# Order of high and low halves around the start of a fused attention and feed-forward kernel: values behind the transposed probabilities, the sixth pair's scores one slot later, the ninth weight behind slot 3

## Chip, cores and metric

One core of a Trainium2 chip. The metric is the device time of the core in microseconds (us), less is better. One launch computes everything.

## The reference

Attention with pooled keys and values (8 batches, 8 heads, 576 positions, head size 64), whose output is laid out as 4608 tokens of 512 and goes through two feed-forward layers (512 to 2048 to 512 each), all in float32:

```python
k_p = k.reshape(B, H, Sp, 8, D).mean(axis=3)
v_p = v.reshape(B, H, Sp, 8, D).mean(axis=3)
attn = softmax(q @ k_p.T / sqrt(D))          # cut
x = attn @ v_p                                # -> 4608 x 512
h = x @ w_in1
g = where(h >= 1, h, where(h <= -1, 0, (h + 1) ** 2 / 4))
x = g @ w_out1
r = maximum(x @ w_in2, 0)
out = (r * r) @ w_out2
```

## The kernel before, in words

Every float32 product is made of three products in a faster type: each operand is split in a high half, rounded on ScalarE, and a low half, the difference, made on VectorE or GpSimd. high x high, high x low and low x high are summed in PSUM. So each operand has two preparing steps (names ending in `_high` and `_low`).

The first part of the kernel goes over 12 chunks of 384 tokens and, in each, over 4 pairs of heads: 48 pairs, called a. For each pair TensorE makes `scores(a)` (L696 on, matmuls L709), VectorE subtracts the row maximum (`below`, L1240 and L1244), ScalarE takes the exponential (`exps`, L954), VectorE normalises (`normal`, L1253 to L1267), TensorE transposes (`transposes`, L722 and L725), ScalarE and VectorE copy out a high and a low half of the transposed probabilities (`probabilities` L960 and L963, `probabilities_low` L1272 and L1276), TensorE multiplies them with the values (`values`, L743 to L746), and the result is split again (`tokens_high`, `tokens_low`, L1283).

Meanwhile the first feed-forward product runs: chunk c has 16 tiles of the hidden dimension, slot g = 16 c + j, one `hidden(g)` of 12 matmuls (L754) in each. Its activation is made by ScalarE (L1073, called relu here, and L1076, the square) and VectorE (L1408, semaphore `g_made`), and stored by SyncE to DRAM through a ring of four tiles `g_st`. relu(g) waits for the store of g - 4. Slots 0 to 3 of the first chunk are done with raw float32 operands (`first_hidden`, L784); hidden(4) is the first split one.

The values of a batch and pair of heads, m, are folded by GpSimd (`fold` L579, `values` L585, L589, L593, giving `v_bd`), ScalarE makes the high half (`values_high`, L989), GpSimd the low ones (`values_low`, L601 and L604). `spread_keys` (L571) places the pooled keys. `v_bd` is one buffer: the last step of `values(m)` waits until `values_low(m - 1)` is done. The 16 tiles of the first weight are split by `weights_high(j)` (L993) on ScalarE and `weights_low(j)` on GpSimd (L610), tiles 4 and 5 on VectorE (L1288).

No planner orders the work: each engine has a list written out by hand, and within it each step waits on semaphores. In the slots a step of a pair stands where `pairs_at(g, step)` puts it (L220 on): steps 0 to 6 are scores; exps and below; normal; transposes; probabilities; values; tokens. Pairs 4 to 7 have a first slot each (1, 4, 7, 9), later ones every fourth slot. In a slot, TensorE does hidden, values, transposes, scores; ScalarE probabilities, tokens_high, relu and square, exps; VectorE probabilities_low, below, tokens_low, normal, and the activation. What GpSimd does before the slots is a straight list (L664 to L686). On ScalarE, `values_high(5..7)` and `weights_high(8..15, 0..3)` stand behind given slots (L1115 to L1123). Pair 5's `scores` also wait for `g_made` 4, since slot 3 used the bank of its output. `hidden(g)` waits for g_made of g - 3 or g - 2 and, in its first round, for its weight's low half.

Before the slots, ScalarE ends its list with exps(4), tokens_first(3) (L969), values_high(4), tokens_high(3); VectorE ends it with weights_low(4), tokens_low(1), weights_low(5), tokens_low(2), tokens_low(3), and then comes the activation of slot 0 and normal(4).

The other parts (a fast product of the block kind for the second, third and fourth feed-forward matrices, L886 and L909) are 75% of the time and not touched.

Of the kernel before, what the change touches and what calls it, by code (L numbers as in the profile page):

```python
# [19 lines left out]
def attention_then_two_ffns(nc, q, k, v, v_rest, w_in1, w_out1, w_in2, w_out2, out, g_dram, y_dram, s_dram):  # L20
# [12 lines left out]


    NC, HP, _, H = q.shape
    B = k.shape[0]
    NF, _, D = w_in1.shape
    S = NC * H // B
    G = S // POOL
# [24 lines left out]
    with ExitStack() as ctx:  # L64
# [139 lines left out]
        def pv_bank(a):  # L204

            return tr_ps[:, P:P + H] if a >= REST_APART and a % 2 else o_ps[:, 0:H]
# [13 lines left out]
        def done(m):  # L220

            return HP * ((S * (m // HP + 1) - 1) // H) + m % HP + 1

        def pairs_at(g, step):

            first = {4: 1, 5: 4, 6: 7, 7: 9}

            def taken_at(a):  # L230
                if a < REST_APART:
                    return first[a] + step
                return 4 * (a - 5) + step + (4 if step > 4 and a % 2 == 0 else 0)

            return [a for a in range(HP, PAIRS) if taken_at(a) == g and (a > HP or step > 2)]
# [17 lines left out]
        def wi_count(j):  # L253

            return (j - FIRST) % NF + 1
# [304 lines left out]
        def _(pool):  # L560
# [5 lines left out]
            def spread_keys(m):  # L566

                pool.wait_ge(k_pooled, m + 1)
                if m >= KRING:
                    pool.wait_ge(s_full, done(m - KRING))  # L570
                pool.tensor_tensor(kT[:, m % KRING, :].rearrange("p (h n) -> p h n", h=2),  # L571
                                   k_pool[m % 2][:, :].unsqueeze(1).broadcast_to([P, 2, G]),
                                   head[:, :].unsqueeze(2).broadcast_to([P, 2, G]), ALU.mult).then_inc(k_ready, 1)

            def fold(m):

                raw = v_raw[m % VRAW]
                pool.wait_ge(v_in[m % VRAW], 64 * (m // VRAW + 1))
                pool.tensor_tensor(raw[:, :, 0:4], raw[:, :, 0:4], raw[:, :, 4:8], ALU.add).then_inc(v_half, 1)  # L579

            def values(m):

                raw = v_raw[m % VRAW]
                pool.wait_ge(v_half, m + 1)
                pool.tensor_tensor(raw[:, :, 0:2], raw[:, :, 0:2], raw[:, :, 2:4], ALU.add).then_inc(v_quarter, 1)  # L585
                pool.wait_ge(v_quarter, m + 1)
                if m:
                    pool.wait_ge(v_spread, m)
                pool.tensor_tensor(v_pool[:, :, :], raw[:, :, 0], raw[:, :, 1], ALU.add).then_inc(v_pooled, 1)  # L589
                pool.wait_ge(v_pooled, m + 1)  # L590
                if m:
                    pool.wait_ge(v_ready, m)
                pool.tensor_tensor(v_bd[:, :, :].rearrange("p m (h d) -> p m h d", h=2),  # L593
                                   v_pool[:, :, :].unsqueeze(2).broadcast_to([P, 2, 2, Dh]),
                                   mask[:, :, :].unsqueeze(3).broadcast_to([P, 2, 2, Dh]), ALU.mult)\
                    .then_inc(v_spread, 1)

            def values_low(m):
                pool.wait_ge(v_hi_ready, m + 1)
                vh, rows = v_hi[m % KRING], slice(64, REST_ROWS)  # L600
                pool.tensor_tensor(v_lo[m % KRING][:, :], v_bd[:, 0, :], vh[:, 0, :].bitcast(F32), ALU.subtract)\  # L601
                    .then_inc(v_low_made, 1)
                pool.wait_ge(v_low_made, m + 1)
                pool.tensor_tensor(vh[rows, 1, :], v_bd[rows, 1, :], vh[rows, 1, :].bitcast(F32), ALU.subtract)\  # L604
                    .then_inc(v_ready, 1)
                pool.wait_ge(v_ready, m + 1)

            def weights_low(j):
                pool.wait_ge(wi_hi_ready, wi_count(j))
                pool.tensor_tensor(wi_lo[j][:, :], wi_raw[j][:, :], wi_hi[j][:, :].bitcast(F32), ALU.subtract)\  # L610
                    .then_inc(wi_ready, 1)
# [44 lines left out]
            for m in range(HP):  # L656
                if m == 1:
                    spread_keys(3)
                fold(m + 1)
                if m in (0, 2):  # L660
                    spread_keys(m + 2)
                values_low(m)
                values(m + 1)
            weights_low(6)  # L664
            values_low(4)
            weights_low(7)
            spread_keys(5)
            fold(5)
            values(5)
            weights_low(8)  # L670
            spread_keys(6)
            values_low(5)
            weights_low(9)
            fold(6)
            values(6)
            weights_low(10)
            spread_keys(7)
            values_low(6)
            weights_low(11)
            fold(7)  # L680
            values(7)
            weights_low(12)
            weights_low(13)
            values_low(7)
            weights_low(14)
            weights_low(15)  # L686
            pool.wait_ge(h_full, FIRST)
            for j in range(FIRST):
                weights_low(j)
# [258 lines left out]
        def _(act):  # L948
            copy = nc.scalar.activation

            def exps(a):
                act.wait_ge(s_below, a + 1)
                probs = prob[a % 2][:, :, :]
                copy(probs, probs, ACT.Exp, scale=Dh ** -0.5 / POOL).then_inc(s_exp, 1)  # L954
# [11 lines left out]
            def tokens_first(a):  # L966

                act.wait_ge(pv_full, a + 1)
                copy(x_first[:, a, :], o_ps[:, 0:H], ACT.Copy).then_inc(x_first_ready, 1)  # L969

            def tokens_high(a):
                c = a // HP
                if c == 0:
                    act.wait_ge(x_first_ready, a + 1)
                    copy(x_hi[0][:, a, :], x_first[:, a, :], ACT.Copy).then_inc(x_hi_ready, 1)
                    return
                act.wait_ge(pv_full, a + 1)
                if c == 1:
                    act.wait_ge(h_full, FIRST)
                    act.wait_ge(x_ready, HP)  # L980
                else:
                    act.wait_ge(h_full, NF * (c - 1))
                copy(x_hi[c % 2][:, a % HP, :], pv_bank(a), ACT.Copy).then_inc(x_hi_ready, 1)

            def values_high(m):
                act.wait_ge(v_spread, m + 1)
                if m >= KRING:
                    act.wait_ge(pv_full, done(m - KRING))
                copy(v_hi[m % KRING][:, :, :], v_bd[:, :, :], ACT.Copy).then_inc(v_hi_ready, 1)  # L989

            def weights_high(j):
                act.wait_ge(weight_in[j], 16)
                copy(wi_hi[j][:, :], wi_raw[j][:, :], ACT.Copy).then_inc(wi_hi_ready, 1)  # L993
# [116 lines left out]
            weights_high(7)  # L1110
            exps(4)
            tokens_first(3)
            values_high(4)
            tokens_high(3)
            for g in range(SLOTS):  # L1115
                slot(g)
                for m, at_slot in ((5, 4), (6, 7), (7, 10)):
                    if g == at_slot:
                        values_high(m)
                for j in {1: (8,), 4: (9,), 5: (10,), 6: (11, 12), 7: (13,), 8: (14,), 9: (15,), 10: (0,), 11: (1, 2),  # L1120
                          12: (3,)}.get(g, ()):
                    weights_high(j)

            for n in range(6, ALL + 4):
# [96 lines left out]
        def _(dve):  # L1221
# [57 lines left out]
            def tokens_low(a):  # L1279
                c, hp = divmod(a, HP)  # L1280
                dve.wait_ge(x_hi_ready, a + 1)
                raw = pv_bank(a) if c else x_first[:, hp, :]
                vec.tensor_tensor(x_lo[c % 2][:, hp, :], raw, x_hi[c % 2][:, hp, :].bitcast(F32),  # L1283
                                  ALU.subtract).then_inc(x_ready, 1)

            def weights_low(j):
                dve.wait_ge(wi_hi_ready, wi_count(j))
                vec.tensor_tensor(wi_lo[j][:, :], wi_raw[j][:, :], wi_hi[j][:, :].bitcast(F32), ALU.subtract)\  # L1288
                    .then_inc(wi_ready_first, 1)
# [172 lines left out]
            probabilities_low(3)  # L1462
            weights_low(4)
            tokens_low(1)
            weights_low(5)
            tokens_low(2)
            tokens_low(3)
            for g in range(-4, SLOTS):
                slot(g)

# [182 lines left out]
```

## Time and profile before

| what | value |
|---|---|
| median of 3 runs | 1573.02 us (1572.12 to 1574.9) |
| the profiled execution's own time | 1574.91 us |
| its span in the profile | 1573.1 us |
| TensorE matmul busy | 1563.8 us (99%) |
| VectorE, ScalarE, GpSimd busy | 1126.4, 831.2, 248.0 us |
| TensorE clock granted | 0.9 or more of full speed in every slice |

The profiler's span runs from the first to the last instruction; all times in the views count from its start. PE is TensorE, DVE VectorE, ACT ScalarE, POOL GpSimd, SP SyncE. In a timeline a row is an instruction, or several alike merged, with its start, its length, what it writes and reads, and in brackets the time that the engine stood idle before it and who released it. A line such as L610 is the line of a helper in the kernel, so tiles are told apart by their order.

### The profile page before, as it was taken

What the parts mean: (1) busy time and instruction counts of PE and PEld (TensorE: products, weight loads), DVE (VectorE), ACT (ScalarE), POOL (GpSimd) and SP (SyncE); (2) the same over time, 40 slices, a digit from 0 to 9 for tenths busy, and PEclk for the clock granted to TensorE, in tenths of its full rate; (3) what the DMA queues carried; (4) which work ended last, traced back from release to release, by engine and by line L of the source; (5) the groups of instructions that cost most, each with busy time, mean ns of one, the idle gap of its engine ahead of it and who ended that gap; (6) DMA issues with size and microseconds to landing.
All of it is one profiled execution on the core that took longest, in us unless ns stands there. A gap on an engine that the chain in (4) does not pass through costs nothing.

```text
span 1573.1 us, 25372 instructions
## 1 busy us (share of the span) xinstructions
PE 1563.8 (99%) x9160; PEld 1545.1 (98%) x9160; DVE 1126.4 (72%) x1823; ACT 831.2 (53%) x1488; POOL 248.0 (16%) x356
## 2 busy tenths in 40 slices
PE   8999999999999999999999999999999999999999
PEld 6999999999999999999999999999999999999999
DVE  7666666667666877877879767667667986876874
ACT  5766668666667544443445654344356643443442
POOL 7655338735500000000000000000000000000000
PEclk9999999999999999999999999999999999999999
DMA  9367479566537444245244642442448645245231
GB/s 292 109 225 226 166 220 326 183 210 228 190 112 244 153 161 152 94 157 164 83 156 169 220 160 101 141 161 103 139 159 289 194 149 195 74 144 186 91 116 41
DMA packets 173950, 262.79 MB, mean 167 GB/s; under 512 B 16640, under 2 KB 153856, under 8 KB 173824
## 3 DMA queue, kind: packets, MB, share of 16 engines
q1 hardware_dynamic: 173824, 261.16, 50.3%
q8 instruction: 73, 1.20, 0.3%
q14 instruction: 53, 0.43, 0.1%
HBM read 154.14 MB, written 106.95 MB: 166 GB/s over the span
## 4 chain that ended last, share of the span: by engine, by line
PE 93%; DVE 3%; ACT 1%; POOL 1%; DMA 1%; issue 1%; SPq 0%; DVEq 0%; POOLq 0%; ACTq 0%
PE bank L886 42%; PE bank L754 24%; PE bank L909 21%; PE bank L709 2%; PE bank L722 1%; DVE gf L1327 1%; DVE b L1320 1%; PE bank L746 1%; PE bank L743 1%; PE bank L744 1%; PE bank L745 1%; DMA f_raw<-moe_w_out 0%; DVE f_lo L1295 0%; ACT pT_rest L963 0%; POOL v_raw L579 0%
## 5 line engine op out<-in xcount | busy, mean ns | idle before, releaser
L886 PE MATMUL bank<-gf,f_hi 128*128 128x384 f32 x2688 | 682.7, 334 | 0.5 <-DVE u_b L1337 0.4
L886 PEld LDWEIGHTS bank<-gf,f_hi 128*128 128x128 f32 x2688 | 485.5, 188 | 1.3 <-DVE u_b L1337 0.9
L886 PE MATMUL bank<-gf,f_lo 128*128 128x384 f32 x1344 | 449.1, 334 | 0.0
L1022 ACT ACTIVATE gf<-b 128x768 fp32r<-128x768 f32 x336 | 278.6, 845 | 264.4 <-PE bank L886 174.1
L1327 DVE TENSOR_TENSOR gf<-b,gf 128x768 fp32r<-128x768 f32 x336 | 314.5, 952 | 43.3 <-ACT gf L1022 43.3
L909 PE MATMUL bank<-xf,w_hi 128*128 128x384 f32 x1344 | 341.6, 335 | 1.0 <-ACT c_st L1154 0.7
L754 PE MATMUL bank<-x_hi,wi_hi 128*128 128x384 f32 x752 | 259.9, 346 | 0.8 <-DVE g_st L1408 0.8
L886 PEld LDWEIGHTS bank<-gf,f_lo 128*128 128x128 f32 x1344 | 252.3, 188 | 0.0
L754 PE MATMUL bank<-x_hi,wi_lo 128*128 128x384 f32 x752 | 252.1, 335 | 0.0
L754 PE MATMUL bank<-x_lo,wi_hi 128*128 128x384 f32 x752 | 252.1, 335 | 0.0
L909 PEld LDWEIGHTS bank<-xf,w_hi 128*128 128x128 f32 x1344 | 242.2, 188 | 2.6 <-ACT c_st L1154 1.7
L909 PE MATMUL bank<-xf,w_lo 128*128 128x384 f32 x672 | 224.6, 334 | 0.0
L1408 DVE SCALAR_TENSOR_TENSOR g_st<-g_st,bank 128x384 f32<-128x384 f32 x192 | 106.0, 553 | 116.6 <-ACT g_st L1076 116.0
L1073 ACT ACTIVATE g_st<-bank,half_sb 128x384 f32<-128x384 f32 x192 | 111.5, 581 | 146.6 <-PE bank L754 142.6
L1320 DVE TENSOR_TENSOR b<-b,b 128x768 f32<-128x768 f32 x192 | 182.3, 952 | 0.0
L754 PEld LDWEIGHTS bank<-x_hi,wi_hi 128*128 128x128 f32 x752 | 141.5, 188 | 1.4 <-DVE g_st L1408 1.4
L754 PEld LDWEIGHTS bank<-x_lo,wi_hi 128*128 128x128 f32 x752 | 141.5, 188 | 0.0
L754 PEld LDWEIGHTS bank<-x_hi,wi_lo 128*128 128x128 f32 x752 | 141.2, 188 | 0.0
L909 PEld LDWEIGHTS bank<-xf,w_lo 128*128 128x128 f32 x672 | 126.2, 188 | 0.0
L1076 ACT ACTIVATE g_st<-g_st 128x384 f32<-128x384 f32 x192 | 101.0, 526 | 6.1
L1154 ACT ACTIVATE c_st<-bank 128x384 f32<-128x384 f32 x48 | 23.3, 486 | 99.6 <-PE bank L909 99.6
L1502 DVE TENSOR_TENSOR u<-bank,p 128x384 f32<-128x384 f32 x48 | 26.7, 557 | 44.0 <-PE bank L909 36.3
(105 smaller groups left out, 1484.5 us busy)
## 6 DMA issues: line engine op xcount, KB each, us to landing
b<-g_dram SPq DMA_DIRECT2D x192, 384.0 KB, 4.4
g_dram<-g_st SPq DMA_DIRECT2D x192, 192.0 KB, 2.4
g_dram<-c_st SPq DMA_DIRECT2D x192, 192.0 KB, 1.9
s_dram<-su_s SPq DMA_DIRECT2D x24, 512.0 KB, 2.9
k_raw<-k SPq DMA_DIRECT2D x32, 288.0 KB, 3.7
q_sb<-q SPq DMA_DIRECT2D x48, 192.0 KB, 3.1
y_dram<-o_st SPq DMA_DIRECT2D x48, 192.0 KB, 2.1
x_raw<-y_dram SPq DMA_DIRECT2D x24, 384.0 KB, 5.3
```

The source lines that it names most:

```text
L709: last = mm(s_ps[a % 2][m0 - t * P:m1 - t * P, t * KEYS:(t + 1) * KEYS], q_sb[a % QRING][:, m0:m1], kT[:, m % KRING, :], start=True, stop= ...
L754: last = mm(h_bank(g)[:, 0:H], w[j][:, cols], x[:, kt, :], start=kt == 0 and n == 0, stop=kt == KT - 1 and n == 2)
L886: last = mm(dst[:, 0:H], w[:, 2 * i + kt, cols], x[:, half, kt, :], start=q_ < 3 and i == 0 and kt == 0 and h == 0, stop=q_ >= 4 and i == ...
L909: last = mm(dst[:, 0:H], w[:, form, cols], x[:, half, kt, :], start=i < 3 and kt == 0 and h == 0, stop=i >= 4 and kt == 1 and h == 2, skip ...
L1022: copy(gf[layer][r % GRING][:, 0], unit_source(n)[:, 2 * i:2 * i + 2, :], ACT.Copy).then_inc(gf_hi, 1)
L1073: copy(g_st[g % GST][:, :], h_bank(g)[:, 0:H], ACT.Relu, bias=half_sb[:, 0:1], scale=0.5)\
L1076: copy(g_st[g % GST][:, :], g_st[g % GST][:, :], ACT.Square).then_inc(act_ready, 1)
L1154: copy(c[:, :], xa_ps[n % 2][:, 0:H], ACT.Relu).then_inc(r11_made, 1)
L1320: vec.tensor_tensor(out_[:, rows, :], first[:, rows, :], other[:, rows, :], ALU.subtract)\
L1327: vec.tensor_tensor(halves[:, 1], unit_source(n)[:, 2 * i:2 * i + 2, :], halves[:, 0].bitcast(F32), ALU.subtract).then_inc(gf_ready, 1)
L1408: vec.scalar_tensor_tensor(h[:, :], h[:, :], 1.0, h_bank(g)[:, 0:H], ALU.min, ALU.max)\
L1502: vec.tensor_tensor(u2[n % 2][:, :], ya_ps[n % 2][:, 0:H], p1[n % 2][:, :], ALU.add).then_inc(u2_made, 1)
```

## The change

It moves steps in three of the hand-written lists and changes one entry of the slot table; no instruction is added or removed.

- TensorE: scores(5) stand in slot 5 instead of slot 4.
- ScalarE: tokens_high(3) before values_high(4). values_high(5), (6), (7) behind slots 5, 8, 11 instead of 4, 7, 10. weights_high(8), (9) behind slot 3 (were behind 1 and 4), (13) behind 8 (was 7), (0) behind 11 (was 10), (1), (2) behind 12 (were 11), (3) behind 13 (was 12).
- VectorE: weights_low(5) behind tokens_low(3) instead of ahead of tokens_low(2).
- GpSimd: values_low(4) before weights_low(6); weights_low(9) before values_low(5); values_low(6) behind fold(7), and values_low(7) behind the last weight.

```diff
@@ pairs_at
             def taken_at(a):
                 if a < REST_APART:
-                    return first[a] + step
+
+                    return first[a] + step + (a == HP + 1 and step == 0)
...
@@ GpSimd
                 values_low(m)
                 values(m + 1)
+            values_low(4)
             weights_low(6)
-            values_low(4)
             weights_low(7)
             spread_keys(5)
             fold(5)
             values(5)
             weights_low(8)
             spread_keys(6)
+            weights_low(9)
             values_low(5)
-            weights_low(9)
             fold(6)
             values(6)
             weights_low(10)
             spread_keys(7)
-            values_low(6)
             weights_low(11)
             fold(7)
+            values_low(6)
             values(7)
-            weights_low(12)
-            weights_low(13)
+            for j in range(12, NF):
+                weights_low(j)
             values_low(7)
-            weights_low(14)
-            weights_low(15)
@@ ScalarE
             tokens_first(3)
+            tokens_high(3)
             values_high(4)
-            tokens_high(3)
             for g in range(SLOTS):
                 slot(g)
-                for m, at_slot in ((5, 4), (6, 7), (7, 10)):
+                for m, at_slot in ((5, 5), (6, 8), (7, 11)):
                     if g == at_slot:
                         values_high(m)
-                for j in {1: (8,), 4: (9,), 5: (10,), 6: (11, 12), 7: (13,), 8: (14,), 9: (15,), 10: (0,), 11: (1, 2),
-                          12: (3,)}.get(g, ()):
+                for j in {3: (8, 9), 5: (10,), 6: (11, 12), 8: (13, 14), 9: (15,), 11: (0,), 12: (1, 2),
+                          13: (3,)}.get(g, ()):
                     weights_high(j)
@@ VectorE
             tokens_low(1)
-            weights_low(5)
             tokens_low(2)
             tokens_low(3)
+            weights_low(5)
```

## Rows read from the trace of the kernel before

**Rows 1.** The page's first part: engine, busy us (share), instructions.
```profile
PE 1563.8 (99%) x9160; PEld 1545.1 (98%) x9160; DVE 1126.4 (72%) x1823; ACT 831.2 (53%) x1488; POOL 248.0 (16%) x356
```

**Rows 2.** Waits of TensorE, whole run: us in total, times, longest.
```profile
PE bank L722 <- DVE prob L1267: 1.5, 5, 0.5
...
PE bank L754 <- DVE g_st L1408: 0.8, 1, 0.8
```

**Rows 3.** Timeline of TensorE, 30 to 63 us: start, length, what.
```profile
30.03 3.59 PE L784 MATMUL bank<-x_first,wi_raw 128*128 128x384 f32 x10
34.43 0.44 PE L754 MATMUL bank<-x_hi,wi_hi 128*128 128x384 f32 x1 [0.81 <-DVE g_st L1408]
...
36.62 0.27 PE L722 MATMUL bank<-ident,prob 128*128 128x128 f32 x1
...
37.52 1.32 PE L709 MATMUL bank<-kT,q_sb 128*128 128x144 f32 x8
...
46.27 0.33 PE L722 MATMUL bank<-ident,prob 128*128 128x128 f32 x1 [0.27 <-DVE prob L1267]
...
60.98 0.34 PE L754 MATMUL bank<-x_hi,wi_lo 128*128 128x384 f32 x1
61.38 0.36 PE L743 MATMUL bank<-pT_hi,v_hi 128*128 128x192 f32 x1
...
62.98 0.33 PE L722 MATMUL bank<-ident,prob 128*128 128x128 f32 x1 [0.46 <-DVE prob L1267]
```

**Rows 4.** The chain that ended last: start, time on the chain, what.
```profile
95.28 6.25 PE bank L754 x36
```

**Rows 5.** Timeline of VectorE, 30 to 43 us.
```profile
30.54 1.10 DVE L1288 TENSOR_TENSOR wi_lo<-wi_raw,wi_hi 128x512 fp32r<-128x512 f32 x1
...
31.56 2.35 DVE L1283 TENSOR_TENSOR x_lo<-x_first,x_hi 128x384 fp32r<-128x384 f32 x2
...
33.83 0.54 DVE L1408 SCALAR_TENSOR_TENSOR g_st<-g_st,bank 128x384 f32<-128x384 f32 x1
...
42.64 0.61 DVE L1240 TENSOR_REDUCE top<-bank 128x6 f32<-128x432 f32 x1
```

**Rows 6.** Tile wi_lo, 0 to 70 us: ns min/median/max, first and last start.
```profile
L610 POOL TENSOR_TENSOR wi_lo<-wi_raw,wi_hi x14: 1274/1290/1715, 31.0 to 65.8; 128x512 fp32r<-128x512 f32 x14
L1288 DVE TENSOR_TENSOR wi_lo<-wi_raw,wi_hi x2: 693/896/1098, 29.2 to 30.5; 128x512 fp32r<-128x512 f32 x2
```

**Rows 7.** Timeline of GpSimd, 30 to 57 us.
```profile
30.27 0.81 POOL L593 TENSOR_TENSOR v_bd<-v_pool,mask 128x256 f32<-128x256 f32 x1
31.05 1.72 POOL L610 TENSOR_TENSOR wi_lo<-wi_raw,wi_hi 128x512 fp32r<-128x512 f32 x1
32.73 0.77 POOL L601 TENSOR_TENSOR v_lo<-v_bd,v_hi 128x128 fp32r<-128x128 f32 x1
...
52.54 0.73 POOL L585 TENSOR_TENSOR v_raw<-v_raw 128x256 f32<-128x256 f32 x1
...
54.46 2.54 POOL L610 TENSOR_TENSOR wi_lo<-wi_raw,wi_hi 128x512 fp32r<-128x512 f32 x2
```

**Rows 8.** Timeline of ScalarE, 30 to 57 us.
```profile
30.23 0.49 ACT L969 ACTIVATE x_first<-bank 128x384 f32<-128x384 f32 x1 [0.29 <-PE bank L746]
...
31.12 0.42 ACT L989 ACTIVATE v_hi<-v_bd 128x256 fp32r<-128x256 f32 x1 [0.40 <-POOL v_bd L593]
...
38.03 0.58 ACT L1073 ACTIVATE g_st<-bank,half_sb 128x384 f32<-128x384 f32 x1 [1.46 <-DMA g_dram<-g_st]
...
39.28 0.42 ACT L989 ACTIVATE v_hi<-v_bd 128x256 fp32r<-128x256 f32 x1
...
40.13 0.47 ACT L960 ACTIVATE pT_hi<-bank 128x384 fp32r<-128x384 f32 x1
...
53.00 0.56 ACT L954 ACTIVATE prob<-prob 128x432 f32<-128x432 f32 x1 [1.30 <-DVE prob L1244]
...
56.52 0.58 ACT L1073 ACTIVATE g_st<-bank,half_sb 128x384 f32<-128x384 f32 x1 [0.52 <-PE bank L754]
```

## The prediction

> **What bounds the kernel now.** I read the page first: TensorE is busy for 1563.8 us of a span of 1573.1 us [rows 1]. So nearly all that a new order can bring is the 9 us in which TensorE stands still, and the next question is where. The waits of TensorE over the whole run answer it: five waits for the normalised probabilities, 1.5 us, and one of a hidden product for the feed-forward activation on VectorE, 0.8 us [rows 2], are the long ones that the change can reach. The timeline of TensorE puts them in the first 63 us [rows 3]; three of the five lie before 30 us, where nothing changes. A matmul of this product is recorded 0.33 us long while the next one follows 0.174 us later (36 in 6.25 us [rows 4]), so an idle time in the timeline is about 0.16 us shorter than the time that the issue was held up. I count hold-ups:
> - hidden(4) starts at 34.43; the raw products before it end at 33.62, so it could start at 33.46: 0.97 us.
> - scores(5) starts at 37.52; the six transposes before it (0.11 us each from 36.62) are issued by 37.28: 0.24 us. It waits for g_made 4.
> - transposes(5) at 46.27, idle 0.27: 0.43 us.
> - values(6) at 61.38, after a matmul issued at 60.98: 0.23 us.
> - transposes(7) at 62.98, idle 0.46: 0.62 us.
> That is 2.49 us, 0.16% of the span. Nothing else in the time that the change touches holds TensorE.
>
> **Part 1: the start (tokens_high(3) before values_high(4) on ScalarE, tokens_low(2), (3) before weights_low(5) on VectorE, values_low(4) before weights_low(6) on GpSimd).** No instruction is added; the gain or loss is in who waits. In the rows VectorE's weights_low(5) takes 1.10 us and the two x_lo behind it 2.35 us, before the activation of slot 0 starts at 33.83 [rows 5]; alone the first of these takes about 0.6 to 0.69, as its sister [rows 6]. On GpSimd the same window holds v_bd to 31.08, weights_low(6) of 1.72 us (its median is 1.29 [rows 6]), then v_lo of 0.77 [rows 7]. The ends alternate: v_bd 31.08, DVE 31.64, POOL 32.77, DVE about 33.1, POOL 33.5, DVE 33.91. Each VectorE instruction that reads two SBUF tensors takes its turn with GpSimd's. So VectorE's start is late mostly by one long turn of GpSimd, weights_low(6).
> New order: x_first(3) ends at 30.72, v_bd at 31.08 [rows 8, 7]. ScalarE does x_hi(3) at about 30.75 to 31.25 (it is as large as x_first, 0.49) and v_hi(4) right behind, done at 31.57 where it was 31.54: no loss. GpSimd has nothing until then, 0.5 us idle. VectorE: x_lo(2) in its turn 31.04 to 31.54, x_lo(3) next to 32.04 (GpSimd asks at 31.64, just too late), v_lo to 32.45, weights_low(5) to 33.0, then the activation at about 32.95 instead of 33.83, whose square from ScalarE is there at 32.6. hidden(4) then starts at 33.55: **0.88 us earlier**. Bounds: if GpSimd's v_lo gets in ahead of x_lo(3), VectorE ends its three 0.46 us later, 0.42 us gained; the upper bound is the 0.97 us. I take 0.88 because the request of VectorE is 0.1 us ahead by the rows.
> Another reading of the same stretched rows is that two engines share the port and both run slower; VectorE then gains only what GpSimd's idle 0.5 us gives back, about 0.55 us. The Trainium skill ("SBUF — State Buffer", section "SBUF: two separate sides") says that the port pair shared by VectorE and GpSimd is an exclusive lock held for a whole instruction, not a split of bandwidth: by that rule the term is 0.88, or 0.42 if the order of arrival flips. With it the trace agrees, in its alternating ends.
> GpSimd ends weights_low(7) and values(5) about 0.45 us later than now. Covered: hidden(6) and hidden(7), which need weights 6 and 7, start near 39.6 and 42.6, some 5 us behind those.
>
> **Part 2: scores(5) one slot later.** TensorE does transposes(4), hidden(5), scores(5), hidden(6). The matmuls are the same. scores(5) no longer stands right behind g_made 4: **0.24 us gained**. What is late next: below(5) on VectorE. It stands behind probabilities_low(4) and started at 42.64 [rows 5], 4.61 behind relu(4); by part 3 that becomes 37.15 + 4.61 - 0.85 = 40.9, and scores(5) is done at about 39.6. Cost nothing; without that cover at most the 1.3 us that scores(5) took [rows 3]. Weights 8 and 9 made on ScalarE behind slot 3 lie in its wait for a store, 1.46 us idle before 38.03 [rows 8]: two of 0.52.
> SyncE issues no transfer at another place. Its loads of q wait for earlier scores only; the next one that counts scores(5) is in slot 9.
>
> **Part 3: values_high(5), weight 9 gone from behind slot 4.** They took 39.28 to 40.13, 0.85 us, right ahead of the copies of the transposed probabilities of pair 4 [rows 8]. The chain relu(4), square, probabilities(4), probabilities_low(4), below(5), exps(5), normal(5), transposes(5) ran from 38.03 to 46.27, 8.24 us; now 7.39. relu(4) is released by the store of activation 0, 4.20 us behind the start of that activation (33.83 to 38.03). From 32.95 that is 37.15, so the probabilities are there at 44.54. TensorE, from hidden(4) at 33.55, needs 46.27 - 34.43 less the 0.24 and 0.43 held up, 11.17 us: it comes at 44.72. The hold-up goes, **0.43 us**, with 0.2 us to spare. Bound: if the store lands at its old time, it is 45.42, a wait of 0.7.
>
> **Part 4: the same for pairs 6 and 7.** values_high(7) and weight 0 leave their place between exps(7) and probabilities(6). The chain from relu(10) at 56.52 to transposes(7) at 62.98 is 6.46 us, less 0.85 is 5.61; TensorE without its hold-ups needs 62.98 - 56.52 - 0.62 - 0.23 = 5.61. So **0.85 us** go, by a hair. If one late copy stays, 0.2 to 0.4 us come back.
>
> **Part 5: GpSimd behind values_high(6).** weights_low(12) now stands behind values_low(6) and values(7). transposes(5) to exps(6) was 46.27 to 53.00, 6.73; 0.84 less for values_high(6) and weight 13: exps(6) starts at 44.72 + 5.89 = 50.6. v_hi(6) is then done at 51.5, values_low(6) (1.0) at 52.6, values(7) (52.54 to 54.46 [rows 7]) at 54.5, weights_low(12) (1.29) at 55.8. hidden(12) starts 12 x 0.174 ahead of 61.15, at 59.07 now, 57.5 then. Spare 1.7 us (it was 3.3). Cost nothing.
>
> **Sum:** 0.88 + 0.24 + 0.43 + 0.85 = 2.4 us. Two of the terms are ties, so I take 2.1 to 2.2. Behind 75 us TensorE waits for other engines only at places that are counted from its own pace, so a head start is kept. The profiled execution took 1574.91 us with a span of 1573.1, and is 1.9 above the median of the three runs, 1573.02. Its span should become 1571.0; against the median that is 1570.9.
>
> **Rivals.**
> - *A half gain.* The lock goes to GpSimd (0.42 for 0.88) or the store lands late (a wait of 0.7 at transposes(5)), or the tie at transposes(7) falls wrong. For it: margins of 0.1 and 0.2 us, DMA traffic in this stretch. Against: the rows put each on the good side. Gain 0.8 to 1.6, 1571.4 to 1572.2.
> - *No change at all.* The waits are only moved: hidden(4) starts earlier, but the probabilities of pairs 5 and 7 are as late as they were (46.2 and 62.9), so TensorE waits there for what it won, and the end is the same: 1573.0. It takes both stores and copies to stay put; relu(4) hanging on a DMA speaks for it, 0.85 us of ScalarE work taken away against it.
> - *Slower: GpSimd's chain becomes the bound at hidden(12).* Place: weights_low(12) behind values_low(6) and values(7), all behind v_hi(6). From v_hi(6) to the end of weights_low(12) is 4.3 us by part 5, so hidden(12) waits as soon as v_hi(6) is done after 53.2. The old run had hidden(12) at 59.07 and lost 0.85 us behind it, so the kernel is slower than before once hidden(12) starts after 59.92, v_hi(6) done after 55.6. If v_hi(6) comes only where v_hi(7) came, done at about 58.4, hidden(12) starts at 62.7, 2.8 us past that point: 1575.8. For it: GpSimd is busy nearly throughout this stretch and now waits for two more copies. Against: v_hi(6) would have to be 4 us behind my count.
> - *The change does more:* a chain freed early makes TensorE's small hold-ups elsewhere in the first 75 us smaller as well. All the waits that are listed there are counted above, so little is left: 1569.8.
>
> **How the numbers follow.** A difference under 0.2%, 3.1 us, can't be told from no change in this kernel. Forecast (gain 1.7 to 2.6) 0.6; half gain 0.2; no change 0.08; slower than before 0.05; more 0.07. Three runs of the same kernel lie 2.8 us apart, so a median may be 1 us off. That gives the forecast case itself about one chance in eight to be read as over 3.1 us faster; with the last case, faster is 0.13; slower by over 3.1 us is 0.03; within is 0.84. The range takes in the half gain and most of no change, and 1.4 us below for the measurement: 1569.5 to 1573.3.
>
> **What would show it.** In the timeline of TensorE: hidden(4) at 33.5 to 33.9 with an idle time under 0.2; transposes(4) followed by hidden(5) and scores(5) without a hold-up; transposes(5) near 44.8 and transposes(7) near 60.7 with none, and hidden(16) some 2.4 us earlier than now. On VectorE three short turns ahead of an activation near 33.0. On GpSimd an idle time of 0.5 us before the v_lo of pair 4. It is wrong if relu(4) still starts at 38.0, if hidden(12) waits for a weight from GpSimd, or if waits of another pair appear.

## The result and the profile after

| | before | after |
|---|---|---|
| median | 1573.04 us (1572.12 to 1574.9, 22 runs) | 1570.65 us (1569.9 to 1572.69, 22 runs) |
| ratio | | 0.9987, 95% interval 0.9981 to 0.9993 |
| span of the profiled execution | 1573.1 us | 1568.5 us |

The kernel is 2.4 us faster, 0.15%, with the interval clear of no change. The spans are 4.6 us apart; the runs below show that some 2.1 of that isn't the change's.

TensorE's busy time in the page of the kernel after (line numbers from here on are those of the kernel that a row comes from: in the kernels made from the new one they are one lower on ScalarE, VectorE and TensorE and one higher on GpSimd and SyncE):

```profile
span 1568.5 us, 25371 instructions
...
PE 1562.2 (100%) x9160; PEld 1545.7 (99%) x9160; DVE 1125.6 (72%) x1823; ACT 831.1 (53%) x1488; POOL 247.7 (16%) x356
```

Its waits over the whole run. The first row is a wait within the first 2 us, the same before. The one for the activation (0.8 us in [rows 2]) is gone; that for the probabilities is 0.9 in 4 instead of 1.5 in 5, and all that is left of it lies before 30 us. At transposes(7) the starts below still show a hold-up of some 0.1 us, too short for an idle time:

```profile
PE bank L804 <- DVE head L1428: 1.1, 1, 1.1
PE bank L721 <- DVE prob L1266: 0.9, 4, 0.3
```

The timeline of TensorE after, at the places of [rows 3]: hidden(4), transposes(4), scores(5), transposes(5), values(6), transposes(7), and hidden(16), which started at 71.86 before. None has an idle time in brackets:

```profile
33.48 0.44 PE L753 MATMUL bank<-x_hi,wi_hi 128*128 128x384 f32 x1
...
35.67 0.27 PE L721 MATMUL bank<-ident,prob 128*128 128x128 f32 x1
...
38.42 1.25 PE L708 MATMUL bank<-kT,q_sb 128*128 128x144 f32 x8
...
44.59 0.30 PE L721 MATMUL bank<-ident,prob 128*128 128x128 f32 x1
...
59.44 0.25 PE L742 MATMUL bank<-pT_hi,v_hi 128*128 128x192 f32 x1
...
60.44 0.33 PE L721 MATMUL bank<-ident,prob 128*128 128x128 f32 x1
...
69.40 0.42 PE L753 MATMUL bank<-x_hi,wi_hi 128*128 128x384 f32 x1
```

The timelines of VectorE, GpSimd and ScalarE after, for [rows 5], [rows 7] and [rows 8]. The three x_lo take 2.17 us together, weights_low(5) 0.94, and the activation of slot 0 starts at 32.87 (33.83 before). GpSimd now does the two steps of values_low(4) first (L602, L605) and weights 6 and 7 after them, in 2.54 us together, no longer stretched; weight 12 starts at 54.72 (the row holds weights 12 to 15). relu(4) starts at 37.38, the high halves of pairs 5 and 6 at 42.69 and 51.25.

```profile
29.77 2.17 DVE L1282 TENSOR_TENSOR x_lo<-x_first,x_hi 128x384 fp32r<-128x384 f32 x3
31.87 0.94 DVE L1287 TENSOR_TENSOR wi_lo<-wi_raw,wi_hi 128x512 fp32r<-128x512 f32 x1
32.87 0.55 DVE L1407 SCALAR_TENSOR_TENSOR g_st<-g_st,bank 128x384 f32<-128x384 f32 x1
```

```profile
31.64 0.62 POOL L602 TENSOR_TENSOR v_lo<-v_bd,v_hi 128x128 fp32r<-128x128 f32 x1 [0.58 <-ACT v_hi L988]
32.34 0.78 POOL L605 TENSOR_TENSOR v_hi<-v_bd,v_hi 32x128 fp32r<-32x128 f32 x1
33.20 2.54 POOL L611 TENSOR_TENSOR wi_lo<-wi_raw,wi_hi 128x512 fp32r<-128x512 f32 x2
...
54.72 5.03 POOL L611 TENSOR_TENSOR wi_lo<-wi_raw,wi_hi 128x512 fp32r<-128x512 f32 x4
```

```profile
37.38 0.58 ACT L1072 ACTIVATE g_st<-bank,half_sb 128x384 f32<-128x384 f32 x1 [0.42 <-DMA g_dram<-g_st]
...
42.69 0.40 ACT L988 ACTIVATE v_hi<-v_bd 128x256 fp32r<-128x256 f32 x1
...
51.25 0.40 ACT L988 ACTIVATE v_hi<-v_bd 128x256 fp32r<-128x256 f32 x1
```

**How the runs are compared.** Whole runs of one kernel spread over 0.8 to 4.1 us and the parts are worth less, so I compare places in the timeline of TensorE. (One of the later executions of the kernel before took 2590.92 us; the medians don't feel it.) The last block of raw products starts at 29.66 to 30.56 us in the profiles (30.03 in [rows 3]), so all is counted from its start to the start of hidden(16): D. It splits in four: raw block to hidden(4); to transposes(5); to transposes(7); to hidden(16).

| kernel | to hidden(4) | to transposes(5) | to transposes(7) | to hidden(16) | D | median us |
|---|---|---|---|---|---|---|
| before | 4.40 | 11.84 | 16.71 | 8.88 | 41.83 | 1573.04 |
| before again (c_before) | 4.65 | 11.85 | 16.71 | 8.86 | 42.07 | 1572.71 |
| after | 3.47 | 11.11 | 15.85 | 8.96 | 39.39 | 1570.65 |
| e_start | 3.46 | 12.92 | 16.71 | 8.87 | 41.96 | 1573.22 |
| e_slots | 4.43 | 11.12 | 15.84 | 8.95 | 40.34 | 1571.43 |
| e_scores | 4.41 | 11.87 | 16.72 | 8.86 | 41.86 | 1572.77 (1 run) |
| e_start5 | 3.47 | 11.50 | 18.21 | 8.86 | 42.04 | 1573.57 |
| e_pool | 4.38 | 11.13 | 15.84 | 8.95 | 40.30 | 1571.29 |
| e_dve | 3.47 | 11.42 | 15.89 | 8.97 | 39.75 | 1570.61 (1 run) |
| e_act | 3.88 | 11.12 | 15.89 | 8.98 | 39.87 | 1570.39 (1 run) |
| e_noscores | 3.79 | 11.42 | 15.84 | 8.98 | 40.03 | 1571.08 |
| e_vh6 | 3.56 | 11.48 | 22.22 | 8.81 | 46.07 | 1576.51 |
| e_vh6_9 | 3.47 | 11.11 | 16.67 | 9.07 | 40.32 | 1571.64 |
| e_forms | 3.47 | 11.15 | 15.88 | 8.97 | 39.47 | 1570.73 |

In D the change is worth 2.44 us, as much as in the medians (2.39).

### The profile page after: what moved, and what is told of

The parts are those of the page before. It is cut to its first block, busy times and chain, and to the rows that moved or that the text cites. A ratio compares the mean times of both kernels' runs of the same rounds, so it can differ in the third digit from the quotient of the medians.

```text
span 1568.5 us, 25371 instructions
## 1 busy us (share of the span) xinstructions
PE 1562.2 (100%) x9160; PEld 1545.7 (99%) x9160; DVE 1125.6 (72%) x1823; ACT 831.1 (53%) x1488; POOL 247.7 (16%) x356
## 4 chain that ended last, share of the span: by engine, by line
PE 96%; DVE 2%; issue 0%; ACT 0%; DMA 0%; DVEq 0%; ACTq 0%
PE bank L885 42%; PE bank L753 25%; PE bank L908 22%; PE bank L708 2%; PE bank L721 1%; DVE gf L1326 1%; DVE b L1319 1%; PE bank L745 1%; PE bank L742 1%; PE bank L743 1%; PE bank L744 1%; PE bank L783 0%; DVE f_lo L1294 0%; PE bank L791 0%; PE bank L724 0%
## 5 line engine op out<-in xcount | busy, mean ns | idle before, releaser
L1352 DVE TENSOR_TENSOR o_st<-bank,u_b 128x384 f32<-128x384 f32 x48 | 26.7, 557 | 41.8 <-PE bank L885 41.0
```

The source lines that it names most:

```text
L1352: vec.tensor_tensor(o_st[layer][o % OUTS][:, :], src[:, 0:H], more[:, :], ALU.add)\
```

## Experiments

### The kernel before, once more, and the parts

**c_before**, no edit.

> The kernel before, unchanged, as a control. The profiles of the two kernels are 4.6 us apart while the medians are 2.4 apart; the first product is 2.5 us ahead at its end, and the other 2.1 us lie between the first and the last matmul of L909 (867.6 to 1219.2 before, 865.2 to 1214.6 after), where ScalarE waits for f_raw from DRAM. Theory A (it belongs to that one execution): this stretch takes 349 to 350 us here and the time is 1573.0. Theory B (it belongs to the old order): 351.6 us again. Both expect hidden(16) to start at 71.9 and a ratio of 1.000.

Measured: ratio 1.0001 (0.9992 to 1.001). The stretch of L909 took 349.1 us (867.9 to 1217.0). The rows of that line, the kernel after first, then the control (count, ns min/median/max, first and last start):

```profile
L908 PE MATMUL bank<-xf,w_hi x1344: 334/334/440, 865.2 to 1214.6; 128*128 128x384 f32 x192
```

```profile
L909 PE MATMUL bank<-xf,w_hi x1344: 334/334/334, 867.9 to 1217.0; 128*128 128x384 f32 x192
```

Theory A holds: of all fourteen profiles of this study the stretch is 349.1 to 349.6 in twelve, 350.3 in e_start's and 351.6 in the first one of the kernel before. So some 2.1 us of the 4.6 belong to that execution, not to its order. The control shows one thing more, which I had not looked for. ScalarE's timeline in it:

```profile
37.20 0.58 ACT L1073 ACTIVATE g_st<-bank,half_sb 128x384 f32<-128x384 f32 x1 [0.40 <-DMA g_dram<-g_st]
...
39.52 0.42 ACT L989 ACTIVATE v_hi<-v_bd 128x256 fp32r<-128x256 f32 x1 [1.18 <-POOL v_bd L593]
```

Here the store landed early and relu(4) started at 37.20 instead of 38.03. It helped nothing: values_high(5) then stood 1.18 us waiting for GpSimd, and transposes(5) came as late as ever (11.85). In this execution GpSimd, not the store, set that chain; e_scores and e_start below show the same.

**e_start**, the start alone:

```diff
 ScalarE   +tokens_high(3) ahead of values_high(4)
 VectorE   +weights_low(5) behind tokens_low(3)
 GpSimd    +values_low(4) ahead of weights_low(6)
 (on the kernel before)
```

> The start alone on the kernel before: tokens_high(3) ahead of values_high(4), weights_low(5) behind tokens_low(3), values_low(4) ahead of weights_low(6). My theory: activation of slot 0 at 32.9, hidden(4) at 33.5 (0.95 earlier); relu(4) near 37.2, so with values_high(5) and weight 9 still in its chain (8.24 us) transposes(5) comes near 45.4 and TensorE waits about 0.5 to 0.7 there; the waits at values(6) and transposes(7) stay. hidden(16) starts at 71.1 to 71.2 instead of 71.9, time 1572.3. Rival 'the parts are independent': the full 0.95 is kept, hidden(16) at 70.9.

Measured: hidden(4) 0.94 us earlier, as expected, and nothing of it left at hidden(16). The ratio is 1.0001 (0.9991 to 1.001). It is worse than my theory: from hidden(4) to transposes(5) takes 12.92, 1.08 more, so all 0.94 are given back. TensorE, then ScalarE:

```profile
34.00 0.44 PE L754 MATMUL bank<-x_hi,wi_hi 128*128 128x384 f32 x1
...
37.69 1.32 PE L709 MATMUL bank<-kT,q_sb 128*128 128x144 f32 x8 [0.68 <-DVE g_st L1408]
...
46.92 0.33 PE L722 MATMUL bank<-ident,prob 128*128 128x128 f32 x1 [0.36 <-DVE prob L1267]
```

```profile
39.93 0.42 ACT L989 ACTIVATE v_hi<-v_bd 128x256 fp32r<-128x256 f32 x1 [0.97 <-POOL v_bd L593]
```

scores(5) still stands behind g_made 4 (idle 0.68), and values_high(5) waits 0.97 us for `v_bd`, which GpSimd, idle 0.6 us at the new start, makes no earlier than before. Both theories fell; e_start5 below takes up the cause.

**e_slots**, all but those three edits:

```diff
 ScalarE   -tokens_high(3) ahead of values_high(4)
 VectorE   -weights_low(5) behind tokens_low(3)
 GpSimd    -values_low(4) ahead of weights_low(6)
 (on the kernel after)
```

> All of the change but the start. My theory: hidden(4) stays at 34.4; scores(5) has no hold-up (0.24), transposes(5) comes near 45.6 without one (0.43), the 0.85 at values(6) and transposes(7) go but for 0.15. hidden(16) starts at 70.4 to 70.5, 1.4 to 1.5 us earlier than before; time 1571.6. Rival 'the moves pay only with the early start': waits stay at transposes(5) and (7), hidden(16) at 71.5 or later.

Measured: D 40.34, 1.49 us less than before; ratio 0.9989 (0.998 to 0.9998). As expected: hidden(4) stays, the hold-ups at transposes(5) and behind go (11.12 and 15.84, the values of the kernel after). So the slots pay by themselves, the start only with them: 0.95 on top of the slots, nothing alone.

**e_scores**, scores(5) alone:

```diff
-                    return first[a] + step
+                    return first[a] + step + (a == HP + 1 and step == 0)
 (on the kernel before)
```

> Only scores(5) one slot later. My theory: the 0.24 hold-up of scores(5) goes, but transposes(5) hangs on relu(4) and the copies behind it and stays at 46.3, with an idle time of about 0.5 instead of 0.27; net nothing, hidden(16) at 71.9. Rival 'scores(5) one slot later gives its 0.24': hidden(16) at 71.6. Rival 'it delays below(5) and so the pair': transposes(5) later than 46.3.

Measured: the expected result. D 41.86; the wait moves to transposes(5), idle 0.36 us instead of 0.27. The reason that I gave is not what the run shows: relu(4) started at 37.55, 0.5 us earlier than before, and transposes(5) came no earlier, because values_high(5) waited for `v_bd` again. TensorE, then ScalarE:

```profile
46.26 0.33 PE L722 MATMUL bank<-ident,prob 128*128 128x128 f32 x1 [0.36 <-DVE prob L1267]
```

```profile
39.28 0.42 ACT L989 ACTIVATE v_hi<-v_bd 128x256 fp32r<-128x256 f32 x1 [0.59 <-POOL v_bd L593]
```

### Where the start's 0.94 us comes from, and the rival

**e_pool**:

```diff
-            values_low(4)
             weights_low(6)
+            values_low(4)
 (GpSimd, on the kernel after)
```

> The kernel after, but with weights_low(6) ahead of values_low(4) on GpSimd again. Measured as D, from the start of the last block of raw products (30.0) to the start of hidden(16): 41.8 before, 39.4 after. Theory 'whole turns': VectorE's three instructions and GpSimd's alternate, x_lo(2), weights_low(6), x_lo(3), v_lo, weights_low(5); the activation of slot 0 starts near 34.35 where it was 32.9, even later than before (33.8), hidden(4) near 34.95, D 40.9. Rival 'both share the port': the same instructions run at the same time as before the change, activation at 33.8, hidden(4) 34.4, D 40.3. Rival 'GpSimd's order is free': 32.9, D 39.4.

Measured: 4.38 us from the raw block to hidden(4), as before the change; D 40.30, ratio 0.9989 (0.9979 to 0.9998). Without GpSimd's one swap the whole gain of the start is gone (the swap alone was not run). The number that came is that of "both share the port", though the rows look like turns. VectorE, then GpSimd (all about 0.4 later than in the kernel after, as the raw block is):

```profile
30.20 3.24 DVE L1282 TENSOR_TENSOR x_lo<-x_first,x_hi 128x384 fp32r<-128x384 f32 x3
33.36 0.94 DVE L1287 TENSOR_TENSOR wi_lo<-wi_raw,wi_hi 128x512 fp32r<-128x512 f32 x1
34.23 0.54 DVE L1407 SCALAR_TENSOR_TENSOR g_st<-g_st,bank 128x384 f32<-128x384 f32 x1
```

```profile
31.45 1.57 POOL L611 TENSOR_TENSOR wi_lo<-wi_raw,wi_hi 128x512 fp32r<-128x512 f32 x1
32.99 0.77 POOL L602 TENSOR_TENSOR v_lo<-v_bd,v_hi 128x128 fp32r<-128x128 f32 x1
```

The mistake was in my sum. Old order and e_pool take the same five turns (weights_low(5), two x_lo, weights_low(6), v_lo) in different sequence, so turns also expect the same end. From the end of v_bd to the end of the fifth they take 33.91 - 31.08 = 2.83 us before and 34.30 - 31.48 = 2.82 here. My sum gave them 3.3 us. Their shortest records in these traces add up to even more, 3.5 us (x_lo 0.55 twice, weights 0.69 and 1.27, v_lo 0.46), so a turn is some 0.1 us shorter than its record. So this run didn't tell the two readings apart. Two things speak against a split of time, short of proof: weights_low(6) took 1.57 us, 1.28 alone, next to a VectorE that had work throughout, and the new order brought 0.93 us at hidden(4), where the prediction's reckoning by a split gave 0.55. The Trainium skill's lock ("SBUF — State Buffer", "SBUF: two separate sides") fits that and the alternating ends; no run here proves it.

**e_dve**:

```diff
+            weights_low(5)
             tokens_low(2)
             tokens_low(3)
-            weights_low(5)
 (VectorE, on the kernel after)
```

> The kernel after, but with weights_low(5) ahead of tokens_low(2) on VectorE again. Theory 'whole turns': weights_low(5) takes the turn up to 31.64, x_lo(2) still gets in ahead of v_lo, x_lo(3) behind it; activation of slot 0 near 33.05, hidden(4) near 33.65, D 39.6: the new order of VectorE is worth under 0.2. Rival 'VectorE's order is what made the start earlier': activation at 33.5 or later, D 40.0 or more.

Measured: 3.47 to hidden(4), the same as after; the new order of VectorE is worth nothing. D is 39.75, 0.36 more, but 0.31 of that lie at transposes(5), because in this execution the store of activation 0, issued at 33.72, released relu(4) only 4.26 us later (3.93 in the kernel after):

```profile
37.98 0.58 ACT L1072 ACTIVATE g_st<-bank,half_sb 128x384 f32<-128x384 f32 x1 [0.76 <-DMA g_dram<-g_st]
```

That is the bound that the prediction gave to its third part: in the new order the store does bind.

**e_act**:

```diff
+            values_high(4)
             tokens_high(3)
-            values_high(4)
 (ScalarE, on the kernel after)
```

> The kernel after, but with values_high(4) ahead of tokens_high(3) on ScalarE again. Theory 'whole turns': x_hi(3) is ready only at 31.95, so v_lo gets its turn ahead of x_lo(3), v_hi ahead of weights_low(5); activation near 33.55, hidden(4) near 34.1, D 40.0 to 40.1. Rival 'ScalarE's order doesn't count, VectorE has weights to do': no change, D 39.4.

Measured: 3.88 to hidden(4), so this swap is worth 0.41 us (0.6 expected). VectorE stands idle for the high half of x:

```profile
31.85 0.56 DVE L1282 TENSOR_TENSOR x_lo<-x_first,x_hi 128x384 fp32r<-128x384 f32 x1 [0.48 <-ACT x_hi L974]
```

**e_vh6**:

```diff
-                for m, at_slot in ((5, 5), (6, 8), (7, 11)):
+                for m, at_slot in ((5, 5), (6, 10), (7, 11)):
 (ScalarE, on the kernel after)
```

> The kernel after, with values_high(6) behind slot 10 instead of 8, to have the slower rival at work. Theory 'GpSimd's list bounds at hidden(12), with 1.7 us to spare': v_hi(6) done at 56.7 instead of 51.7, weights_low(12) done 4.3 later at 61.0 where hidden(12) wants it at 57.4; TensorE waits 3.6 there, and the hold-up of 0.15 at transposes(7) goes. D 42.8, time near 1574.0, slower than before. Rival 'GpSimd has slack everywhere': D 39.4 to 39.8.

Measured: 1576.51 us, ratio to the kernel before 1.0021 (1.0012 to 1.0031), D 46.07. The wait is the expected one, 3.66 us idle before hidden(12), a hold-up of 3.83, right behind GpSimd's weight 12, the first of the four in GpSimd's row (60.30 to some 61.57; the profile names VectorE as releaser, long done). But the price is 6.7 us in D, and 5.9 between the medians, not 3.4. TensorE's timeline, GpSimd's row, and the windows (after the stretch: busy us of PE, PEld, DVE, ACT, POOL, the granted clock, DMA share, GB/s):

```profile
61.71 0.66 PE L753 MATMUL bank<-x_hi,wi_hi 128*128 128x384 f32 x1 [3.66 <-DVE g_st L1407]
62.17 0.53 PE L753 MATMUL bank<-x_lo,wi_hi 128*128 128x384 f32 x1
62.49 0.53 PE L753 MATMUL bank<-x_hi,wi_lo 128*128 128x384 f32 x1
```

```profile
60.30 4.97 POOL L611 TENSOR_TENSOR wi_lo<-wi_raw,wi_hi 128x512 fp32r<-128x512 f32 x4
```

```profile
59.00:61.00 2.00, 0.00 (x0) 0.00 (x0) 1.88 (x6) 1.22 (x4) 1.84 (x4) 0.85 0.00 0
61.00:62.00 1.00, 0.29 (x1) 0.32 (x2) 0.68 (x2) 0.31 (x1) 1.00 (x2) 0.50 0.00 0
...
66.00:68.00 2.00, 2.00 (x15) 1.96 (x15) 0.55 (x1) 1.97 (x4) 1.82 (x3) 0.69 0.03 8
68.00:70.00 2.00, 2.00 (x16) 2.00 (x15) 0.46 (x1) 1.91 (x5) 2.00 (x2) 1.00 0.62 177
```

The granted clock falls to 0.50, the 1.2 GHz level, while TensorE stands still, and stays there up to some 67.2 us (0.69 is the mean over 66 to 68): matmuls follow each other in 0.32 us, not 0.174. hidden(12) takes 3.98 us (61.71 to 65.69) where it takes 2.1, values(6) 1.6 instead of 1.0: 2.5 us more. The rest of D lies ahead of it and is not the wait's: 0.37 at transposes(5) by a late store (4.34 us from its issue to relu(4)) and 0.09 at hidden(4).

### What held the start, the scores, and a short wait

**e_start5**:

```diff
-                for m, at_slot in ((5, 4), (6, 7), (7, 10)):
+                for m, at_slot in ((5, 5), (6, 7), (7, 10)):
-                for j in {1: (8,), 4: (9,), 5: (10,), ...
+                for j in {3: (8, 9), 5: (10,), ...
 (ScalarE, on e_start)
```

> The start as in the run with the start alone (which gained nothing, D 42.0), and with it values_high(5) behind slot 5 and weights 8, 9 behind slot 3; scores(5) and pairs 6 and 7 stay as before. Theory 'GpSimd held ScalarE': in the start alone v_bd of pair 5 was done only at 39.9, ScalarE stood 0.97 us in front of values_high(5) and the copies of pair 4 behind it came late. Without it in the way transposes(5) comes 11.1 to 11.4 behind hidden(4) without a wait, the 0.85 behind it stays: D 40.4 to 40.6, time 1571.6. Rival 'the store binds': transposes(5) still waits 0.4 or more, D 41.2 or more.

Measured: the cause holds, its result doesn't. transposes(5) comes without idle time, 11.50 behind hidden(4) instead of 12.92: it was GpSimd that held ScalarE. But D is 42.04. The same wait turns up a pair later. GpSimd, with values_low(5) still ahead of weights_low(9), now stands 2.26 us for v_hi(5); `v_bd` of pair 6 is late, ScalarE waits for it 1.75 us in slot 7, and TensorE 1.26 us at values(5):

```profile
48.60 0.42 ACT L989 ACTIVATE v_hi<-v_bd 128x256 fp32r<-128x256 f32 x1 [1.75 <-POOL v_bd L593]
```

```profile
51.98 0.36 PE L743 MATMUL bank<-pT_hi,v_hi 128*128 128x192 f32 x1 [1.26 <-DVE pT_rest L1276]
```

So the move of pair 5 doesn't pay without more of the change. Whether it takes the moves of pairs 6 and 7, or only GpSimd's weight 9 ahead of values_low(5), no run here separates. The ratio is 1.0006 (0.9997 to 1.0015); its median, 0.9 us over that of the kernel before run beside it, is more than D says (0.2). D comes from the fastest of its ten executions; the cause of the rest is open.

**e_noscores**:

```diff
-                    return first[a] + step + (a == HP + 1 and step == 0)
+                    return first[a] + step
 (on the kernel after)
```

> The kernel after, with scores(5) back in slot 4. My theory: the activation of slot 3 is done at 36.5, the transposes at 36.3, so scores(5) is held up 0.25 and all behind it comes 0.25 later, less what transposes(5) had to wait anyway: D 39.5 to 39.65 (39.4 after), time 1570.8. Rival 'early scores help the chain of pair 5': D 39.4 or less. Rival 'the move is what makes the gain': D 40.5.

Measured: from hidden(4) to transposes(5) 11.42 instead of 11.11, so the move of scores(5) is worth 0.31 us in the new order (0.1 to 0.25 expected) and nothing in the old. TensorE was held up some 0.24 us in front of scores(5), the starts say, and reached transposes(5) without a wait, so a late store has no part in this. D, 40.03, holds another 0.32 from the start, where v_bd and v_hi(4) came about 0.4 us later in this execution.

**e_vh6_9**:

```diff
-                for m, at_slot in ((5, 5), (6, 8), (7, 11)):
+                for m, at_slot in ((5, 5), (6, 9), (7, 11)):
 (ScalarE, on the kernel after)
```

> The kernel after, with values_high(6) behind slot 9 instead of 8. v_hi(6) done at 54.1, weights_low(12) at 58.4, wanted at 57.4: TensorE waits 1.0 at hidden(12). Theory 'a short wait costs only itself' (0.8 us in the kernel before left the clock at 1.00): D 40.2 to 40.4, time 1571.5. Rival 'a wait here takes the clock too', as the 3.7 us did (granted 0.50 for the next 5 us, 2.6 us more): D 42 to 43, time 1573.5.

Measured: D 40.32 and 1571.64 us, both as expected of the short wait. TensorE's row and the window:

```profile
58.10 0.41 PE L753 MATMUL bank<-x_hi,wi_hi 128*128 128x384 f32 x1 [0.66 <-POOL wi_lo L611]
```

```profile
57.00:59.00 2.00, 1.34 (x8) 1.05 (x7) 1.40 (x3) 1.93 (x6) 2.00 (x2) 1.00 0.28 102
```

The clock stays at 1.00 (2.4 GHz) after 0.66 us, and the wait costs itself.

**e_forms**, a try at the spread of the runs:

```diff
-{"0A": range(4), "0B": range(4, 8), "2B": range(8, 12)}
+{"0B": range(4), "0C": range(4, 8), "2B": range(8, 12)}
 (high halves of the last product's forms, ScalarE, on the kernel after)
```

> The kernel after, with the first eight high halves of the last product's forms one place later on ScalarE (0B and 0C instead of 0A and 0B), where they no longer stand in front of evictions while their loads are under way. Theory: the stretch of L909 takes 349.1 in most executions and up to 351.6 in some, by a load that lands late; with the move it is 349.1 always, the median 0 to 0.3 us lower (1570.4 to 1570.6) and the highest run no more than 1571.5. Rival 'the spread has another source': median and highest run stay, 1570.7 and 1572.5. Rival 'the halves are then late for VectorE': slower.

Measured: 1570.73 us, 11 runs from 1570.11 to 1570.93; the stretch of L909 349.1. The highest run is as low as expected, the median isn't lower than that of the kernel after (its stretch was 349.4 in the profile). The kernel after wasn't run beside it, so whether the narrow spread is the move's isn't settled. No kernel here beats the one after clearly.

## Why the prediction was right, and where it wasn't

**The forecast** was 1570.9 us (1569.5 to 1573.3), no difference of over 3.1 us with 0.84; measured 1570.65. The gain, 2.39 in the medians and 2.44 in D, is that of the full sum, 2.4, not of the 2.1 to 2.2 taken after it for two ties. The span of the profiled execution is 1568.5 where 1571.0 was said; some 2.1 of these 2.5 us are the stretch of L909 in the profile before, which the prediction took for the kernel's own. In the profile each landmark is within 0.3 us: activation of slot 0 at 32.87 (32.95 said), hidden(4) 33.48 (33.55), relu(4) 37.38 (37.15), transposes(5) 44.59 (44.72), v_hi(6) done at 51.65 (51.5), weights_low(12) done near 56.0 (55.8), transposes(7) 60.44 (60.7).

**Part 1** held in size: 0.93 us to hidden(4) for 0.88. The runs say what does it: taking back GpSimd's swap costs 0.91 (e_pool), ScalarE's 0.41 (e_act; either undoes part of the same gain, so they don't add), VectorE's nothing (e_dve). The prediction listed VectorE's order among the causes without a price of its own; next to the other two it has none. That turns, and not a split, make the stretching is likely but not shown.

**Part 2** held: 0.24 said, 0.31 measured with the rest in place. It didn't say that this alone gives nothing, which e_scores shows.

**Part 3 named the wrong bound for the old order.** It started the chain of pair 5 at relu(4), released by a store, and got the right length, because in the profiled execution the two ends met: values_high(5) started at 39.28, when `v_bd` was done at 39.25 and the square of slot 4 at 39.17. GpSimd, then ScalarE, in the kernel before:

```profile
38.64 0.61 POOL L593 TENSOR_TENSOR v_bd<-v_pool,mask 128x256 f32<-128x256 f32 x1
```

```profile
38.64 0.53 ACT L1076 ACTIVATE g_st<-g_st 128x384 f32<-128x384 f32 x1
```

c_before, with relu(4) 0.8 us earlier and transposes(5) no earlier, and e_scores, with 0.5, show that GpSimd bound. The error would have cost the forecast of the start alone, and did, in e_start's expectation.

In the new order the chain does start at the store. Two of its terms were off against each other. From relu(4) to transposes(5) it is 7.21 us (7.18 in e_dve), 0.18 less than the 7.39 said: with values_high(5) and weight 9, some 0.2 us by which values_high(5) started after the square went too. And relu(4) was 0.23 later than said. It does not follow the activation of slot 0 as the prediction had it. Counted from the raw block it starts 7.14 to 8.00 us later in the five profiles with the slow start (median 7.57; 8.00, the latest of all, is the one that the prediction read), and 7.28 to 7.87 in the nine with an earlier one (median 7.50), though the store is issued 0.5 to 1.2 us earlier there. In the kernel after it was 7.37, which makes the tie that the forecast needed; 7.71 and 7.87 cost 0.31 and 0.37 us (e_dve, e_vh6). So the 0.43 us came out as said, but with some luck in the store. Why an earlier issue doesn't bring an earlier landing, no run here shows.

**Part 4** held: 0.86 us between transposes(5) and (7), 0.85 said. **Part 5** held: weight 12 with 1.4 us to spare (56.0 against hidden(12) near 57.4), 1.7 said, and e_vh6 and e_vh6_9 show the price past that point.

**The rivals.** A half gain did not come in the median, though its parts, a late store (e_dve, 0.3 us at transposes(5)) and a later start (e_noscores, 0.32), come in single executions. "No change" is what the start without the slots gives. The slower rival has its place and its point right and its price too low: hidden(12) at 61.71 (e_vh6) is 1.8 us past the 59.92 at which it saw the kernel level with the one before, and the medians are 3.5 apart. It left out the clock, 2.5 us on top of the hold-up of 3.8.

## What to carry over

When an order of queues is changed, price each part also without the others: here the start alone, the scores alone, and the start with one pair moved each gained nothing, because every wait taken away reappeared one step or one pair further on. In a chain, look for the second waiter that ends within 0.1 us of the first; a second profile of the same kernel shows it. A wait on a store is to be read from several profiles as well: one of them said nothing of how the landing would move. And take a difference of two profiles apart by stretches before it is put down to the change: 2.1 of 4.6 us was one execution's.

## What the runs showed of the hardware

- In an idle time of TensorE of 3.66 us (e_vh6) the granted clock fell to 0.50 and was 1.00 again only at some 67.2 us, 5.5 us after the work went on, with 2.5 us lost on top of the wait; idle times of 0.66 (e_vh6_9), 0.81 (before), 1.06 (c_before) and 1.26 us (e_start5) left it at 1.00.
- From the issue of the same store to the instruction that it released took 2.57 us (c_before) to 4.34 (e_vh6) in the fourteen profiles; 3.63 before and 3.93 after. A store issued 0.5 to 1.2 us earlier released relu(4) at about the same time: 7.50 us behind the raw block in the median, 7.57 with the late issue.
- Five instructions of VectorE and GpSimd with two SBUF inputs each, 3.5 us by their shortest records, ended in 2.82 to 2.83 us in either sequence, one after the other.
